# Interleaved attention and expert layers on one core: an earlier query load, another order of low weights, masks and value sums, a layer-1 step ahead of a task's transposes, and a finer wait

## The reference

```python
scores_l = where(|i - j| < 16, scale * q k^T, -1e9)
scores_s = scale * q (max of each 32 keys)^T + log(32)
a = softmax(concat(scores_l, scores_s)); x = a @ concat(v, mean of each 32 values)
x = sum over e < 4 of p[:, e] * (relu(x @ w1[e]) @ w2[e])     # dense experts, p from domain_probs
y = x + gate * (relu(x @ v1[best]) @ v2[best])   where x @ w_skip > 0, else x   # 8 experts, one for each row
```

## Time and profile before

| | us |
|---|---|
| median of 3 runs | 795.9 (795.27 to 798.83) |
| the profiled execution | 797.93 |
| span of its instructions | 796.2 |
| TensorE busy (matmuls) | 757.3 |
| VectorE busy | 350.6 |
| ScalarE busy | 261.7 |
| GpSimd busy | 77.7 |
| mean granted TensorE clock | 0.985 of full |

### The profile page before, as it was taken

How to read it: one execution, slowest core, us unless ns; L and a number is a source line. 1 busy time by engine, 2 the same in 40 slices (tenths; PEclk the granted TensorE clock), 3 DMA queues, 4 the chain that set the end, 5 groups by cost and what they waited for, 6 DMA issues and landing times.

```text
span 796.2 us, 12799 instructions
## 1 busy us (share of the span) xinstructions
PE 757.3 (95%) x4516; PEld 664.8 (83%) x4517; DVE 350.6 (44%) x818; ACT 261.7 (33%) x572; POOL 77.7 (10%) x119
## 2 busy tenths in 40 slices
PE   4679989999999999999999999999999979999996
PEld 4568888888998989989899898998989857788885
DVE  4966664452432212234112133323232569972982
ACT  3744444351320101123011031220202237753861
POOL 2521000000000000000000000000010125233121
PEclk9899999999999999999999999999999989999999
DMA  9974722112221000033000003220203347972830
GB/s 200 201 179 94 146 51 58 36 38 104 87 75 54 1 0 0 0 106 106 0 0 0 0 2 130 80 80 1 80 1 133 107 164 243 386 284 100 284 147 17
DMA packets 77483, 75.05 MB, mean 94 GB/s; under 512 B 54644, under 2 KB 54900, under 8 KB 77056
## 3 DMA queue, kind: packets, MB, share of 16 engines
q1 hardware_dynamic: 74224, 69.82, 29.1%
q0 software_dynamic: 3216, 4.66, 1.9%
HBM read 68.30 MB, written 9.29 MB: 97 GB/s over the span
## 4 chain that ended last, share of the span: by engine, by line
PE 88%; DVE 4%; DMA 3%; ACT 2%; issue 2%; SPq 1%; ACTq 0%; POOL 0%; DVEq 0%; POOLq 0%
PE ps L1194 22%; PE ps L1196 22%; PE ps L1195 22%; PE ps L1486 2%; PE ps L1490 2%; PE ps L1495 2%; PE ps L1464 2%; PE ps L1456 2%; PE ps L1471 2%; PE ps L1228 1%; PE ps L1256 1%; PE ps L1376 1%; DMA stage<-in_q 1%; PE ps L1445 1%; DMA acc<-in_moe_w 1%
## 5 line engine op out<-in xcount | busy, mean ns | idle before, releaser
L666 ACT ACTIVATE h_hi<-ps 128x384 fp32r<-128x384 f32 x128 | 63.0, 492 | 367.6 <-PE ps L1196 367.5
L1194 PE MATMUL ps<-xt_hi,w_hi 128*128 128x384 f32 (+1 forms) x508 | 174.2, 343 | 2.1 <-issue 2.0
L1195 PE MATMUL ps<-xt_lo,w_hi 128*128 128x384 f32 (+1 forms) x508 | 171.1, 337 | 0.0
L1196 PE MATMUL ps<-xt_hi,w_lo 128*128 128x384 f32 (+1 forms) x508 | 171.0, 337 | 0.0
L1194 PE MATMUL ps<-w_hi,h_hi 128*128 128x512 f32 x384 | 151.8, 395 | 0.0
L1196 PE MATMUL ps<-w_hi,h_lo 128*128 128x512 f32 x384 | 149.9, 390 | 0.0
L902 DVE SCALAR_TENSOR_TENSOR h_lo<-ps,h_hi 128x384 fp32r<-128x384 f32 x128 | 71.3, 557 | 178.4 <-ACT h_hi L666 178.3
L1195 PE MATMUL ps<-w_lo,h_hi 128*128 128x512 f32 x384 | 149.9, 390 | 0.0
L1194 PEld LDWEIGHTS ps<-xt_hi,w_hi 128*128 128x128 f32 x508 | 96.2, 189 | 4.4 <-issue 3.7
L1195 PEld LDWEIGHTS ps<-xt_lo,w_hi 128*128 128x128 f32 x508 | 96.3, 190 | 0.5
L1196 PEld LDWEIGHTS ps<-xt_hi,w_lo 128*128 128x128 f32 x508 | 96.3, 190 | 0.0
(11 more groups left out here) (187 smaller groups left out, 805.8 us busy)
## 6 DMA issues: line engine op xcount, KB each, us to landing
stage<-in_moe_w SPq DMA_DIRECT2D x56, 512.0 KB, 5.0
acc<-in_moe_w SPq DMA_DIRECT2D x36, 512.0 KB, 5.6
stage<-in_k SPq DMA_DIRECT2D x16, 192.0 KB, 4.4
acc<-in_v SPq DMA_DIRECT2D x4, 768.0 KB, 6.9
x_rows<-acc SPq DMA_DIRECT2D x4, 768.0 KB, 3.6
out_rows<-acc SPq DMA_DIRECT2D x4, 768.0 KB, 5.2
acc<-in_moe_w POOLq DMA_DIRECT2D x4, 512.0 KB, 4.4
v_all<-in_v SPq DMA_DIRECT2D x16, 120.0 KB, 3.4
```

The lines of the kernel that those rows point to most:

```text
L666: nc.scalar.activation(h_hi[:, f, :], ps[:, f % 2, 0:GT], ACT.Relu).then_inc(h_hi_ok, 1)
L1194: mm(dst, a_hi, b_hi, start=start, stop=False)
L1195: mm(dst, a_hi, b_lo, start=False, stop=False)
L1196: return mm(dst, a_lo, b_hi, start=False, stop=stop)
```

## The change

Five edits of order, with the same work in all of them. On SyncE the load of queries 6 goes behind that of queries 5. On VectorE the low weights 2 and 3 go ahead of `mask(4, 0)`, with `low_o(3)` between them. `sum_values(3)` goes from step f = 3 to step f = 2. On TensorE, in task 4 alone, the second step (f = 1) goes ahead of `turn(4, 0)`. And a group's wait for the low parts of its inputs is taken slice by slice in the loop over `kc`.

```diff
--- before.py
+++ after.py
@@ -336,6 +336,7 @@
             load_windows(2)
             load_windows(3)
             load_queries(5)
+            load_queries(6)
             sp.dma_start(dp[:, :, :], dprobs.rearrange("(t p) e -> p t e", p=P)).then_inc(dp_in, 16)
             first_w2(0)
             first_w2(1)
@@ -343,7 +344,6 @@
             load_sums(4)
             load_values(2)
             first_w2(2)
-            load_queries(6)
             load_windows(5)
             load_sums(5)
             first_w2(3)
@@ -929,9 +929,10 @@
             norm(3, 1)
             low_w1(0, early_w1, [1])
             low_o(2)
+            low_w1(0, early_w1, [2])
+            low_o(3)
+            low_w1(0, early_w1, [3])
             mask(4, 0)
-            low_o(3)
-            low_w1(0, early_w1, [2, 3])
             mask(4, 1)
             norm(4, 0)
 
@@ -953,7 +954,7 @@
                         low_w2(0, f // 2, early_w2(f // 2))
                     if c == 0 and f == 6:
                         shares()
-                    if c == 1 and f == 3:
+                    if c == 1 and f == 2:
                         sum_values(3)
                     yield
                 for j in range(2 * GR):
@@ -1275,10 +1276,13 @@
                         transpose_keys(a + 1)
                     transpose_queries(a + 1)
                 fill(0)
+                if a == LEAD:
+                    fill(1)
                 turn(a, 0)
                 if more:
                     qk(a + 1)
-                fill(1)
+                if a > LEAD:
+                    fill(1)
                 turn(a, 1)
                 fill(2)
                 pv(a)
@@ -1307,11 +1311,11 @@
                     yield
                 else:
                     pe.wait_ge(w1_ok, PIECES * e + PIECES)
-                    if first:
-                        pe.wait_ge(o_lo, PAIRS * (c + 1))
                 for f in range(1 if first and c == 0 else 0, FC):
                     pe.wait_ge(h_ok, FC * c + f + 1)
                     for kc in range(KC):
+                        if first and f == 0:
+                            pe.wait_ge(o_lo, PAIRS * c + kc + 1)
                         cols = (slice(None), bass.ds(PAIRS * b + kc, 1), slice(half * GT, half * GT + GT))
                         w = (slice(None), kc, slice(f * P, (f + 1) * P))
                         last = three(ps[:, f % 2, 0:GT], w1_hi[w], w1_lo[w],
```

## The result

The changed kernel takes 786.1 us (median of four, 785.8 to 787.4), the kernel before 796.3 in the same runs: a ratio of 0.987, with a 95% interval of 0.985 to 0.990. It is faster by 10.2 us. Forecast were 783.3 and a gain of 12.6. A second set of six runs gave 785.8 and 0.986 (0.984 to 0.989). One execution of the kernel before, in the set of the first undoings, took 2631.5 us at a granted clock of 1.00, and it is left out of every figure; why it took so long is not known.

What follows compares the result with a forecast made beforehand. TensorE, busy 757.3 of 796.2 us, bounds the kernel; only idle and low-clock time can return. 4.1 (queries 6) + 1.7 (task 4) + 4.1 (value sums) + 2.7 (slices) = 12.6: median 795.9 to 783.3, range 781.5 to 785.5, wide to 787.5.

Steps and rivals of the forecast that it cites:

- value sums: Before scores(10): summing one step earlier removes 2.6 us of wait and 1.55 of low clock, together 4.1 us.
- slices: Starts of groups 1, 2 and 3: waiting slice by slice gains 0.34, 1.05 and 1.30, together 2.7 us.
- task 4: Early low weights and step 1 ahead of turn(4, 0): pv(4) at 50.95, step 3 at 51.8 for 53.48; 1.7 us.
- queries 6: Load issued behind queries 5: TensorE's 2.40 us wait before their transposes and the low clock behind it go; 4.1 us.
- the wide one: Range up to 787.5 us, given 8 in 10, covering the forecast and most of the load, task 4 and keys 10 rivals.
- rivals of task 4: Contention or a slower chain: the edits of task 4 give nothing or cost half a microsecond; 785 to 785.5 us; 10%.
- keys 10: Rival before scores(10): keys late all the same, a microsecond or two of wait remains, clock falls; 786.4 us; 5%.
- a late load: Rival: queries 7 or sums 5 find DMA engines full, TensorE waits again in task 5 or 6; 787.4 us; 11%.
- What I take back is more than the wait: At the transposes of queries 6: besides 2.40 us of wait, 0.15 of draining and 1.55 of low clock return; 4.1 us.
- residual wait: Before scores(10), with the sums moved: TensorE ready at 110.2, keys at 110.3 or 110.4; 0.1 to 0.2 us remain.
- slower rival: Task 4's chain stays late, gaps of some 2 us in each task, low clock through group 0; about 803 us; 3%.
- rival of contention: In task 4: GpSimd's w2 cast falls onto norm(4, 0), or the chain is slower; 785 to 785.5 us; 10%.

Runs made afterwards that it cites:

- the fillers: Changed kernel plus transposes of the identity, computing nothing used, in TensorE's waits before turn(1, 0), turn(2, 0) and turn(3, 1): 789.0 us, ratio 0.991.

## Why the prediction was right, and where its sizes were not

The direction held, and so did the mechanism of the value sums, the slices and task 4: the waits they were to remove are gone and come back when the edit is undone. For queries 6 the mechanism was that of one profile. The point was 2.8 us too low. The 786.1 lie above the forecast's own range (781.5 to 785.5), and inside the wide one, to 787.5, which had been opened for the rivals of task 4, keys 10 and a late load. None of these came about, so the upper part of the range held in part by luck.

Of the signs named, most came: no wait at the transposes of queries 6, 0.2 us ahead of scores(10) at a clock of 1.00, none ahead of groups 2 and 3, pv(4) at 51.59 for 51, layer 2 of group 0 at 67.46 for 66.9. A sign of being wrong was touched: the clock was 0.50 until 44.6 us, where the text wanted no such stretch from 44 on.

- **Queries 6.** The term that failed is "What I take back is more than the wait": 2.40 + 0.15 + 1.55 = 4.1 us. It is right for the one profile it came from. As the change stands the early load is worth 0.6 us by the medians and 0.2 by the ratios, which the runs do not tell from nothing, and at most 1.8 on the kernel before. The traces show two reasons. The wait was 2.40, 0.77 and 0 in three profiles, for its two ends move on their own: the load by when SyncE issues it (48.67, 50.56, 49.10), TensorE by its clock and its waits ahead of it (there at 55.8, 58.3 and 59.3). And the low weights, by releasing SyncE two microseconds earlier, mend the load too. I had written the second down ("released earlier by about 2 us, because low weight 2 is") and did not apply it to queries 6 themselves.
- **Task 4.** 1.7 was predicted; 1.04 by the one trace, 2.9 by undoing both edits (2.4 by the ratios). The trace compared a profile of before whose clock was full at 42 to 54 us with one of after whose clock was at 0.78 up to 47.8. The chain was read rightly: norm(4, 0) was forecast to end at 46.2 and ended at 46.93, pv(4) was forecast for 50.95 and came at 51.59. Both are late by about the 0.7 by which pv(3) ended late, 0.4 of it for the clock and 0.3 for a later start.
- **Both together**, by the front of three profiles before and of five whose front is the changed one (57.04, 57.96, 56.96, 57.26 and, with the fillers, 57.06): 61.84 to 57.26, 4.6 us, against 5.8 predicted. Behind the front it is 733.4 to 727.3 by three profiles before and two of the changed kernel, 6.1 us, against 6.8 predicted.
- **Value sums.** 4.1 predicted, 4.2 measured by undoing (3.7 by the ratios), 4.1 by the trace. The residual wait of 0.1 to 0.2 was 0.2. But the 1.55 us for the clock were the middle of something between 0 and 2.45.
- **Slices.** 2.7 predicted from issue times, 2.3 in the trace for groups 2 and 3 and 0.3 for group 1, 2.0 by the medians.
- **From one profile to the median.** "It stood 2.0 us above the median of the runs. So the median goes from 795.9 to 783.3." That step failed. Some of the 2.0 us must have been part of what was counted as gain, waits and fallen clocks that other executions have in smaller size; the three profiles of before show it for the wait for queries 6. The profile's gain, 12.1, was forecast well at 12.6; the median's is 10.2. The four undoings of load, task 4, sums and slices add to 0.6 + 2.9 + 4.2 + 2.0 = 9.7, and to 8.8 by the ratios.
- **Two sums that do not come out.** The lower end of the range, 781.5, is 0.5 us below what its named terms give (783.3 - 0.55 for task 4 - 0.1 for the slices - 0.6 of spread = 782.05). The 803 of the slower rival does not follow from its terms either: 21 us on 795.9, less the 10.9 of the other edits, are 806.0.
- **The rivals.** In neither profile of the changed kernel was a load late behind 42 us; queries 7 went out at 57.8 and 59.5, and nobody waited. The rival of contention did not come about as told. The cast of w2 piece 1 ran at 46.89, as norm(4, 0) ended, and not on it. By the rule of the Trainium skill that was cited ("GPSIMD Engine Reference", Key points) this edit was to give 1.2 instead of 1.7. The trace neither bears that out nor speaks against the rule, for the cast and norm(4, 0) did not meet. The cast fell beside norm(4, 1), whose first instruction, at 47.50, took 0.46 us instead of 0.17; turn(4, 1) followed at 49.03 without idle time.

How much of the time of the fallen clock in one place is handed to the next was seen in traces of single executions; which of these the median execution resembles is not settled.

## What to carry to other kernels

A term read from one profile is one draw. Before a stall and the clock behind it go into a sum, ask whether its two ends are set by the same thing. Where one is a DMA's landing and the other TensorE's arrival, its length changes more from one execution to the next than the time at its end does (2.4 us against 0.7 here), and it belongs in the sum at a part of its length. When two edits release the same queue, price each with the other in place: here either removed the late load.

## What the runs showed that I had not expected

After the same idle time of 2.70 or 2.71 us on TensorE, in the same place, the granted clock in the stretch behind was 1.00 in one execution and 0.50, 0.50, 0.62 and 0.65 in four others. At turn(4, 0) two waits lie close together, and their sum did not tell the clock behind them either: 1.95 and 2.03 us were followed by 1.00, 1.82 by 0.64, and 2.56 by 0.52 in one execution and 0.62 in another. So the idle time before a stretch did not by itself tell its clock. This alone makes 0 to 2.45 us for one wait, a quarter of the whole gain. A second source of scatter lies ahead of all this: pv(3) waited for a load for 0.66 to 1.76 us in six of the fourteen profiles and not at all in the others. And the kernel before varied more (793.7 to 799.7 us over all its runs but the one of 2631.5) than any one of the edits gains.
